# Attention with two expert stages: the expert layers rewritten as wide block products

## The reference

```python
def _attn_ref(q, k, v):                    # q, k, v: 4 x 8 x 576 x 64
    scores = scale * np.matmul(q, k.transpose(0, 1, 3, 2))
    mask = block_i >= block_j              # blocks of 64
    ...
    return np.matmul(attn, v).astype(np.float32)

def _moe_ref(x, domain_probs, w1, w2):     # x 2304 x 512, w1 4 x 512 x 1024, w2 4 x 1024 x 512
    p = domain_probs / (domain_probs.sum(-1, keepdims=True) + 1e-09)
    for e in range(E):
        h = np.maximum(x @ w1[e], 0.0)
        out += p[:, e:e + 1] * (h @ w2[e])

def _moe2_ref(x, w_in, w_out, g_ln):
    h = x @ w_in
    h_max = np.max(h, axis=-1, keepdims=True)
    e = np.exp(h - h_max)
    solu = h * (e / (np.sum(e, axis=-1, keepdims=True) + 1e-09))
    ...
    ln = (solu - mu) / np.sqrt(var + 1e-06) * g_ln
    return ln @ w_out
```

## Time and profile before

| | |
|---|---|
| Median of 3 runs | 1148.3 us (1147.96 to 1150.5) |
| Span of the profiled execution, first to last instruction | 1147.4 us |
| TensorE, its weight loads | busy 99%, 89% of the span |
| VectorE, ScalarE, GpSimd | busy 55%, 37%, 36% |
| Granted TensorE clock | 1.000 |

### The profile page before, as it was taken

One profiled execution on the slowest core, in us unless ns is written; L12 is line 12 of the kernel. 1 busy time (PEld: TensorE's weight loads), 2 busy tenths in 40 slices (PEclk: granted clock), 3 DMA queues, 4 the chain that ended last, 5 costly groups with the idle time before them and its releaser, 6 DMA issues.

```text
span 1147.4 us, 16738 instructions
## 1 busy us (share of the span) xinstructions
PE 1134.8 (99%) x6115; PEld 1019.1 (89%) x6115; DVE 632.1 (55%) x1139; ACT 429.7 (37%) x943; POOL 418.4 (36%) x402
## 2 busy tenths in 40 slices
PE   8999999999999999999999999999999999999998
PEld 7999998888899998899999889999988987888887
DVE  8999996443343534244533334443424478667765
ACT  7998985312233211123211113321112354433432
POOL 8999996618144000034300004400003463533330
PEclk9999999999999999999999999999999999999999
DMA  4766768974825031253304071504125100000001
GB/s 153 230 214 218 238 195 259 363 290 168 319 65 217 13 133 60 83 202 119 130 19 175 1 265 56 212 1 150 44 89 196 44 12 10 29 19 28 19 28 37
DMA packets 68342, 146.29 MB, mean 128 GB/s; under 512 B 6064, under 2 KB 34736, under 8 KB 68272
## 3 DMA queue, kind: packets, MB, share of 16 engines
q1 hardware_dynamic: 67840, 145.29, 36.2%
q10 hardware_dynamic: 432, 0.07, 0.0%
HBM read 114.60 MB, written 30.74 MB: 127 GB/s over the span
## 4 chain that ended last, share of the span: by engine, by line
PE 89%; DMA 4%; POOL 2%; DVE 2%; ACT 1%; issue 1%; SPq 0%; DVEq 0%; ACTq 0%; POOLq 0%
PE s L1749 36%; PE outp L1612 19%; PE s L1612 15%; PE ring L1612 11%; PE ring L1623 3%; DMA x_stash<-x_tmp 2%; PE outp L1656 2%; PE outp L1655 2%; PE ring L1880 1%; DMA xr<-x_stash 1%; POOL x_tmp L781 1%; PE s L1823 1%; DMA q_raw<-in_q 1%; DVE neg_max L1232 1%; DMA x_rows<-x_n 0%
## 5 line engine op out<-in xcount | busy, mean ns | idle before, releaser
L1749 PE MATMUL s<-xr,w1s 128*128 128x384 f32 x2016 | 359.4, 336 | 3.9 <-DMA xr<-x_stash 1.8
L1749 PEld LDWEIGHTS s<-xr,w1s 128*128 128x128 f32 x2016 | 350.6, 188 | 8.7 <-DMA xr<-x_stash 2.1
L1082 ACT ACTIVATE hid_h<-u 128x384 fp32r<-128x384 f32 x96 | 50.5, 526 | 370.3 <-DVE u L1435 344.5
L716 POOL TENSOR_TENSOR work<-work 128x256 f32<-128x256 f32 x20 | 14.8, 738 | 392.0 <-DMA work<-in_moe_w 267.1
L1390 DVE SCALAR_TENSOR_TENSOR hid_l<-s,hid_h 128x384 fp32r<-128x384 f32 x48 | 26.8, 558 | 125.1 <-ACT hid_h L1078 125.1
L1348 DVE TENSOR_TENSOR u<-s,m_b 128x384 f32<-128x384 f32 x24 | 13.4, 558 | 132.0 <-PE s L1749 132.0
L1749 PE MATMUL s<-w1s,yop_h 128*128 128x512 f32 x252 | 85.2, 399 | 0.3 <-issue 0.3
L1078 ACT ACTIVATE hid_h<-s 128x384 fp32r<-128x384 f32 x48 | 23.6, 491 | 155.3 <-PE s L1612 155.3
L918 ACT ACTIVATE pr<-s,neg_max 128x576 f32<-128x576 f32 (+2 forms) x144 | 76.2, 541 | 4.4 <-DVE neg_max L1232 2.2
L1612 PE MATMUL s<-k_h,qb 128*128 128x288 f32 (+8 forms) x320 | 76.1, 325 | 1.8 <-DVE k_l L1244 1.1
L1612 PE MATMUL outp<-w_h,hid_h 128*128 128x512 f32 x192 | 75.5, 393 | 0.0
(11 more groups left out here) (169 smaller groups left out, 2444.0 us busy)
## 6 DMA issues: line engine op xcount, KB each, us to landing
xr<-x_stash SPq DMA_DIRECT2D x77, 768.0 KB, 6.1
r_sb<-r_scratch SPq DMA_DIRECT2D x16, 576.0 KB, 4.3
x_rows<-x_n SPq DMA_DIRECT2D x32, 288.0 KB, 4.5
work<-x_rows SPq DMA_DIRECT2D x24, 384.0 KB, 5.7
x_stash<-x_tmp SPq DMA_DIRECT2D x12, 768.0 KB, 3.7
work<-in_moe_w SPq DMA_DIRECT2D x32, 256.0 KB, 3.9
stage<-in_moe_w SPq DMA_DIRECT2D x32, 256.0 KB, 5.3
x_stash<-xr SPq DMA_DIRECT2D x7, 768.0 KB, 9.5
```

What stands on the lines that cost most here:

```text
L716: pool.tensor_tensor(s1, a21, a22, ALU.add).then_inc(w1_sums, 1)
L1082: act.activation(hid[slot][0][:, :], source, ACT.Relu).then_inc(hid_high, 1)
L1749: last = pe.matmul(target, x, y, start=start and i == 0, stop=stop and i == 2, skip_group_check=True)
```

## The change

The experts are reorganised in 12 phases (4 experts x 3 groups of 768 tokens). In a phase TensorE does `up` for all seven products in turn, each over the whole hidden width, then `down` for seven products. The second layer is now computed transposed: `w2` blocks (sums too, of the same seven-product form) are the weights, 384 tokens are the moving columns. Both layers have 7 x 24 = 168 matmuls of 384 columns per phase.

- VectorE and ScalarE collect the first layer's products in SBUF blocks h11, h12, h22, h21 (`copy_product`, `add_product`), and Relu and the share are applied there (`fold`, `last_block`), so that the share is in the operand.
- The sums T1 to T4 of hidden blocks are made on VectorE (`make_t1`, `make_t2`) and GpSimd (`make_t3`, `make_t4`). `operand_high` and `operand_low` split the 14 operands of a phase, 768 columns each, into three spare buffers.
- After each product of the second layer VectorE adds PSUM into `acc` (`flush`), a buffer for one token group. y is kept in DRAM (`y_rows`): `load_acc`, `store_acc`.
- The operands of x come from `x_stash` through a ring of five buffers of 768 columns (`load_ring`), 14 loads per phase, also for the first group, whose operands are stored during attention (`stash_first`).
- The weight blocks of a layer are made in one go of 1024 columns (`w_difference`, `w_low_part` on GpSimd, `cast_w` on ScalarE): the next expert's first layer in its predecessor's last phase, the second layer in the expert's own first phase.
- `turn_y` goes; y is loaded from DRAM (`load_y`). `w_out` is split in eight pieces at the end of the experts (`cast_out`, `out_low`).
- In `last_step` of attention `first_up` takes the place of `up(0, ...)`, in halves.

```diff
             def last_step(p, par):
                 turn(T8, p, par)
                 turn(T8R, p, par)
                 values_left(p - 1)
-                up(0, "m1")
+                first_up("m1", 0)
                 turn(T67, p, par)
+                first_up("m1", 1)
                 turn(T67B, p, par)
...
+            def up(n, name):
+                k, e = ORDER.index(name), n // SUPERS
...
+                for t in range(2):
+                    g = 2 * k + t
+                    b = tuple(grain_of(ring_x[ring_seat(n, g)], low) for low in range(2))
+                    pe.wait_ge(ring_loaded[ring_seat(n, g)], 16 * ring_turn(n, g))
+                    for u in range(HALF_F):
+                        if t == 0 and u % 2 == 0:
+                            bank_free(n, name, u // 2)
+                        last = up_product(k, name, u, t, b)
...
+            def down(n, name):
+                k, e = ORDER.index(name), n // SUPERS
+                if n % SUPERS == 0:
+                    pe.wait_ge(w_low, NP * job2(e) + k + 1)
...
+                if name in ("m6", "m7", "m3", "m4"):
+                    pe.wait_ge(flush_done, flushed(n, {"m6": "m1", "m7": "m6", "m3": "m5", "m4": "m7"}[name]))
+                for h in range(2):
+                    pe.wait_ge(op_low, operand_no(n, name, h))
+                    part = spare[(2 * NP * n + 2 * k + h) % SPARE]
+                    for u in (2 * h, 2 * h + 1):
...
+                        for c in range(2):
+                            last = sharing(bank_down(name, c), (w2_of(k, 0, u, c), w2_of(k, 1, u, c)), b,
...
+            for n in range(PHASES):
+                if n >= 1:
+                    for name in ORDER:
+                        up(n, name)
+                for name in ORDER:
+                    down(n, name)
...
+            def fold(n, block, after, h):
...
+                dve.scalar_tensor_tensor(out=half_rows(target, h), in0=half_rows(target, h), scalar=0.0, in1=share_of(j),
+                                         op0=ALU.max, op1=ALU.mult).then_inc(folded, 1)
...
+            def make_t2(n, h):
+                dve.wait_ge(t1_made, halves(n, h))
+                dve.wait_ge(folded, folded_no(n, "h22", 1))
+                if h:
+                    dve.wait_ge(t4_made, halves(n, 0))
+                    dve.wait_ge(op_low, operand_no(n, "m6", 0))
...
+            def operand_low(n, g):
...
+                dve.tensor_tensor(part[:, PAIR_COLS:2 * PAIR_COLS], t2[:, :] if source is None else half_of(source, h),
+                                  part[:, 0:PAIR_COLS].bitcast(f32), ALU.subtract).then_inc(op_low, 1)
...
+            def first_layer(n):
+                if n >= 1:
+                    flush(n - 1, "m4")
+                for h in range(2):
+                    add_product(n, "m2", h, h11)
...
+                for h in range(2):
+                    fold(n, "h11", "m2", h)
+                if n >= 1:
+                    operand_low(n, 0)
+                    operand_low(n, 1)
+                    for h in range(2):
+                        add_product(n, "m7", h, h22)
...
+                    for h in range(2):
+                        fold(n, "h22", "m7", h)
+                for h in range(2):
+                    add_product(n, "m3", h, h12)
+                for h in range(2):
+                    fold(n, "h12", "m3", h)
+                if n >= 1:
+                    for h in range(2):
+                        make_t1(n, h)
+                for h in range(2):
+                    last_block(n, h)
...
+                else:
+                    operand_low(n, 2)
+                    make_t2(n, 0)
+                    operand_low(n, 3)
+                flush(n, "m1")
+                if n >= 1:
+                    operand_low(n, 4)
+                make_t2(n, 1)
...
+                operand_low(n, 5)
+                flush(n, "m2")
+                operand_low(n, 6)
+                operand_low(n, 7)
...
+            for n in range(1, PHASES):
+                e, sg = n // SUPERS, n % SUPERS
+                job = job1(e + 1) if sg == SUPERS - 1 else job2(e) if sg == 0 and e >= 1 else None
...
+                elif job is None:
+                    make_t4(n, 0)
+                    make_t3(n, 0)
+                    make_t4(n, 1)
+                    make_t3(n, 1)
+                else:
+                    w_difference(job, 0)
+                    w_difference(job, 1)
+                    w_low_part(job, A11)
+                    w_difference(job, 2)
+                    w_low_part(job, A12)
+                    w_low_part(job, S2)
...
+                    w_low_part(job, S1)
+                    w_low_part(job, S3)
...
+                    w_difference(job, 3)
+                    w_low_part(job, S4)
+                    if sg == 0:
+                        w_low_part(job, A22)
+                    if n > 2:
+                        make_t4(n, 0)
+                        make_t3(n, 0)
...
             for p in range(TP - 1):
                 hidden(p, "m1")
-                if p == 0:
-                    turn_y(1)
```

More of the change, by code:

```diff
@@ L124, in next_w2, with order_up, upped @@
[L124 to L134, removed]
+    RING = 5
+    SPARE = 3
+    def order_up(n):
+        return FIRST_ORDER if n == 0 else ORDER
+    def upped(n, name, u=HALF_F - 1):
+        return NP * HALF_F * n + HALF_F * order_up(n).index(name) + u + 1
@@ L656, in _ @@
[L656 to L666 removed]
+                    sp.dma_start(g_col[:, :], g_ln).then_inc(gains_loaded, 16)
@@ new lines, in _ @@
+            sp.dma_start(p_dram.rearrange("e (t x) -> t e x", t=TT), probs_raw[:, :].rearrange("t (e x) -> t e x", e=EXPERTS)
+                         ).then_inc(shares_stored, 16)
+            store_x(PAIRS - 1)
+            load_raw(job2(0), (3,))
+            stash_late(0, 0)
+            load_share(0)
+            stash_late(0, 1)
+            stash_late(0, 2)
+            for k_ in range(3, NP):
+                stash_late(0, k_)
+            load_late(1)
+            for k_ in range(NP):
+                stash_late(1, k_)
+                if k_ == 3:
+                    load_late(2)
+                if k_ in (4, 5):
+                    load_ring(1, k_ - 4)
@@ new lines, in _ @@
+            for g in range(2, RING):
+                load_ring(1, g)
+            load_share(1)
+            store_acc(0, ACC11)
+            load_ring(1, 5)
+            store_acc(0, ACC22)
+            load_ring(1, 6)
+            stash_late(2, 0)
+            load_ring(1, 7)
+            stash_late(2, 1)
+            stash_late(2, 2)
+            store_acc(0, ACC12)
+            load_ring(1, 8)
+            store_acc(0, ACC21)
+            load_ring(1, 9)
+            stash_late(2, 3)
+            load_ring(1, 10)
@@ new lines, in _ @@
+            stash_late(2, 4)
+            load_ring(1, 11)
+            load_ring(1, 12)
+            stash_late(2, 5)
+            load_ring(1, 13)
+            stash_late(2, 6)
+            load_late(3)
+            load_ring(2, 0)
+            store_acc(1, ACC11)
+            load_share(2)
+            stash_late(3, 0)
+            load_ring(2, 1)
+            load_ring(2, 2)
+            stash_late(3, 1)
+            load_ring(2, 3)
+            load_ring(2, 4)
+            for k_ in range(2, 5):
+                stash_late(3, k_)
```

1694 lines of the change are left out of this document (1012 added, 682 removed).

## The result

The changed kernel takes 1228.6 us (median of 4 runs, 1226.5 to 1232.1) beside 1148.9 us of the kernel before: ratio 1.0693, 95% interval 1.0673 to 1.0713. It is slower, as the likeliest case (A) had it; 1210 was forecast. The profiled execution has a span of 1226.4 us.

A forecast was written before the change was run, and what follows sets the result against it. TensorE was taken to bound the kernel. Start of phase 1 at 268 plus 737 us for phases 1 to 11 gave 1005, +72; with -3 for the rest, span 1216, less 6: 1210 us, range 1120 to 1245.

The forecast's parts named there:

- likeliest case (A): Expert phases: VectorE and GpSimd take turns at the SBUF port and stall TensorE; 1180 to 1245 us, likeliest 1210, chance 0.50.
- TensorE's arithmetic: Expert phases: 336 matmuls of 384 columns at 173.5 ns take 58.3 us instead of 61.9, 3.6 us less per phase.
- The port: Expert phases: VectorE operations with two SBUF operands and GpSimd's run one after the other; 24 of 39 new operations are such.
- Rival (C): Expert phases: port waits stay inside VectorE's 24 us of slack per phase; 1117 to 1139 us with small stalls, chance 0.27.
- The stalls: TensorE's waits for `operand_low`: 5.3 us in plain phases, 10.7 or 10.8 in those with weight work.
- The walk with every meeting going badly: Queues followed from a phase start, each port meeting causing its delay: phases of 63.6, 69.0 and 69.1 us.
- Phases 1 and 2: First two phases after the start: 62 us, with late token sums on GpSimd, and 70 us, with weight work.
- rival (D): SyncE's single queue delays ring loads by 2 to 5 us per phase on top; above 1245 us, chance 0.06.
- The start and the tail: Phase 1 starts at 268 us instead of 251.5; behind the experts +1 and -4.4 us as y's transposes go.
- the walk without the port: Phase 0 followed without port turns: lower bound of 252.5 us for its end; 268 to 272 with turns taken.
- The subtraction: Whole kernel: 6 us taken off the span of 1216 because some meetings might just miss, giving 1210.
- The signs by which to judge: Matmul pitch 173.5 ns; low parts and folds 1.3 us or more, flushes near 0.95; TensorE idle 5 or about 10 us.

The follow-up runs named there:

- the memset runs: Changed kernel with GpSimd's later weight operations as memsets, 1174.8 us; GpSimd-narrow kernel with unneeded GpSimd work, memsets in phase 10, 1143.4 us.
- the subtractions that nobody waits for: Changed kernel with GpSimd's sums and weight operations narrow, plus eight unneeded 1024-column GpSimd subtractions in phase 4: 62.9 us for that phase, 1143.4 in all.
- the faster m2: Changed kernel with 40 or 32 small transposes on TensorE ahead of m2 of `down` in phases 3, 5, 6, 8, 9, 11: 1235.3 us.

## Why the prediction was right, and where its sizes were off

**TensorE's arithmetic.** Right. With GpSimd's work made small, phases take 58.8 us against 61.9 before. The 3.6 us per phase were 3.1: 24 matmuls of `down` start 4.16 us apart, those of `up` 4.24 (in the chain of waits), 176.7 ns each and not 173.5. Half a microsecond per phase, 6 us in all, was mis-sized. The columns do pay. The Trainium skill, "TensorE: Matmul & The Clock Gate", section "Back-to-back issue gap", gives sustained spacings of 81 ns at 128 and 131 ns at 512 columns. By an estimate from them the columns would not pay; the 173.3 ns at 384 columns in `down` here (4.16 us for 24) contradict them, as the earlier trace rows do.

**The port.** Right, and the step on which everything hung. Rival (C), in which the waits stay in VectorE's slack, is out: the plain phases alone take 5.4 us above 58.3. Three things are now shown and were only argued. The turns need GpSimd's reads: low parts under memsets take 0.95 us. They need two SBUF operands on VectorE's side: flushes stay at 0.95. And they need no wait for GpSimd's results, as the subtractions that nobody waits for show. The Trainium skill, "SBUF — State Buffer", section "SBUF: two separate sides", says that the two-input VectorE operation is locked out only against a GpSimd operation that reads SBUF; the memset runs agree, by 955 ns each and low parts of 0.95 under them.

**The stalls.** The walk with every meeting going badly came out right, phase by phase, to within 1.1 us in phases 3 to 11 (604.1 us for 605.1), but for that it owes something to luck. The meetings and their order were right; the waits were over-forecast by a third, 80.4 us for 51.8. Low part 2 was late by 5.97 us in phases 3, 6 and 9 (7.2 forecast) and by 4.4 in phases 5, 8 and 11 (5.0), low part 5 of a plain phase by 2.11 (2.6). What made up for it was not in my sum: TensorE was busy for 27.6 us more than 9 x 58.3. Some 4.5 us of that are the pitch of `up`, and some 14 are matmuls behind a wait that ran at a lower granted clock; the other 9 I cannot place. Behind the waits of 4.4 and 6.0 us ahead of m2 the granted clock was 0.58 to 0.72, and 24 matmuls took 5.97 to 7.14 us for 4.3. Behind 2.11 us it was 0.61 in phase 4 (3.58 us for 2.3), but 1.00 in phases 7 and 10, with the same wait:

```profile
724.47 2.38 PE L2276 MATMUL ring<-spare,w2s 128*128 128x384 f32 x12 [2.11 <-DVE spare L1859]
```

**Phases 1 and 2.** Mis-sized, by 3.8 and 7.0 us. I had costed ring loads at nothing there. They were late by 2.4 us in phase 1 and by 1.0, 1.4 and 1.4 in phase 2, where the raw weights share the queue: rival (D)'s mechanism, in two phases out of eleven. Phase 2's low part 2 was 5.4 us late besides, with 6.85 us for m2.

**The start and the tail.** Phase 1 starts at 269.9 (268), and the tail gained 5.1 us (3.4). The run with memsets in phases 0 to 2 puts the start at 253.3; the lower bound by the walk without the port was 252.5.

**The subtraction.** The sum of these steps was a span of 1216. Then I took off 6 us because meetings might just miss. This was the one step with no row behind it. The waits were indeed shorter than in the walk, but not the phases, as the slower matmuls took that back. From 1210 to 1228.6: 6 for the subtraction, 11.8 for the end of the experts (1016.8 for 1005), -1.7 for the tail, 2.2 for the median above the profiled span, and 0.3 of rounding. Likeliest case and range held it.

**The signs by which to judge.** The ones that tell the theories apart came: low parts (1.27 us in the mean over the whole trace) and folds (1.63) well over 0.95 us, flushes near it, TensorE's idle time named after `operand_low` and longest before m2. In size three fell short: 1.27 is under the 1.3 named for low parts, the pitch of `up` is 176.7 ns and not 173.5, and TensorE is idle for 2.8 to 3.8 us in plain phases and 5.2 to 8.1 in those with weights, not 5 and about 10.

## What to carry to other kernels

Before VectorE is given operations with two SBUF operands beside GpSimd that reads SBUF, add the two engines' times and not the larger of them, and price each meeting on a chain of explicit waits by the whole GpSimd operation; an operation moved from GpSimd to VectorE can shorten the phase though VectorE is the busier of the two. Walk the queues of one phase, and afterwards check its parts and not only its sum: here waits forecast 28 us too long and slower matmuls left out cancelled each other. Make no correction by feeling; the one made here cost 6 of the 18.6 us. When an experiment removes a stall, look at the next wait before booking the gain: the faster m2 gave nothing.

## What the runs showed of the hardware

- GpSimd over 1024 columns: a subtraction of two operands took 2.4 us, a copy 1.04 at the shortest, a memset 0.955. Beside VectorE's low parts the copies took 1.65 us in the median, the memsets 0.956.
- With low parts waiting all the time, VectorE and GpSimd alternate one for one: a subtraction every 2.57 us, a low part in each.
- A wait of TensorE of 2.1 us was followed by 12 matmuls at 298 ns instead of about 190 each in phase 4 (granted clock 0.61), and by 12 at full speed in phases 7 and 10 (1.00). One of 6.0 us was followed by 24 at 272 instead of 180 (0.64). With small transposes in that wait the granted clock stayed at 1.00. What decides between the two outcomes behind 2.1 us was not tried.
- 24 matmuls of 384 columns start 4.16 us apart in `down` and 4.24 in `up`, in the phases without waits. Why the two differ was not tried.
